# An mLSTM, soft-MoE and SoLU kernel: gate terms kept in one run for each head and chunk, and weights fetched from ScalarE's queue

## The reference, cut to what matters

```
m_new  = maximum(f_gate[t] + m, i_gate[t])
f_stab = exp(f_gate[t] + m - m_new);  i_stab = exp(i_gate[t] - m_new)
C = f_stab * C + i_stab * outer(v[t], k[t]);  n = f_stab * n + i_stab * k[t]
y[t] = sigmoid(o_gate[t]) * (C @ q[t]) / maximum(|n . q[t]|, 1)
```

## Time and profile before

| | |
|---|---|
| median of 3 runs | 301.03 us (300.47 to 301.7) |
| the profiled execution, its own time | 300.29 us |
| its span in the profile | 298.5 us |
| mean granted TensorE clock over the span | 0.966 |
| TensorE matmul busy | 277.6 us, 93% |
| VectorE, ScalarE, GpSimd busy | 223.2, 212.1, 152.1 us |
| moved by DMA | 50.35 MB |

### The profile page before, as it was taken

How to read it: one execution, slowest core, us unless ns; L and a number is a source line. 1 busy time by engine, 2 the same in 40 slices (tenths; PEclk the granted TensorE clock), 3 DMA queues, 4 the chain that set the end, 5 groups by cost and what they waited for, 6 DMA issues and landing times.

```text
span 298.5 us, 10417 instructions
## 1 busy us (share of the span) xinstructions
PE 277.6 (93%) x3909; PEld 189.0 (63%) x3934; DVE 223.2 (75%) x459; ACT 212.1 (71%) x675; POOL 152.1 (51%) x210
## 2 busy tenths in 40 slices
PE   8796999999989999999899989999999999999985
PEld 3464888888878888886315434666566666656653
DVE  7668557988878989875671048888988989889872
ACT  8675557786878787854117114798988989889895
POOL 2348447666767674455200602365464654646544
PEclk9999559999999999999989999999999999999999
DMA  5998985979989897999497000001010110101102
GB/s 144 270 274 194 350 298 159 319 211 307 311 247 303 225 317 213 369 393 379 161 431 315 0 2 0 2 24 45 24 47 22 47 46 24 46 25 46 45 24 88
DMA packets 22345, 50.35 MB, mean 169 GB/s; under 512 B 5944, under 2 KB 15128, under 8 KB 20120
## 3 DMA queue, kind: packets, MB, share of 16 engines
q1 hardware_dynamic: 22296, 49.70, 50.5%
HBM read 44.04 MB, written 4.18 MB: 162 GB/s over the span
## 4 chain that ended last, share of the span: by engine, by line
PE 50%; ACT 20%; issue 9%; DVE 9%; SPq 6%; DMA 3%; POOL 2%; DVEq 0%; POOLq 0%; ACTq 0%
PE ps L691 7%; ACT ring L1295 7%; ACT ring L1283 7%; PE ps L706 6%; PE ps L1014 6%; PE ps L901 4%; DVE ring L1609 4%; PE ps L937 3%; PE ps L786 3%; PE ps L773 2%; ACT ring L1262 2%; PE ps L676 2%; DMA kept_dram<-ring 2%; PE ps L977 2%; DMA arena<-kept_dram 1%
## 5 line engine op out<-in xcount | busy, mean ns | idle before, releaser
L1014 PE MATMUL ps<-arena,ring 128*128 128x321 bf16 x576 | 87.9, 301 | 1.0 <-DVE ring L1649 1.0
L633 POOL TENSOR_TENSOR ring<-ring 128x1024 bf16<-128x1024 f32 x23 | 43.6, 1896 | 59.7 <-DVE ring L1649 53.9
L1014 PEld LDWEIGHTS ps<-arena,ring 128*128 128x128 bf16 x576 | 54.3, 98 | 26.0 <-issue 4.4
L1295 ACT ACTIVATE ring<-ps,ring 128x256 f32<-128x256 f32 x96 | 44.2, 472 | 18.2 <-DVE ring L1666 18.2
L1324 DVE TENSOR_TENSOR ps<-ps,arena 128x512 f32<-128x512 f32 x48 | 33.2, 699 | 21.7 <-PE ps L691 15.0
L1083 ACT ACTIVATE arena<-ps 128x512 f32<-128x512 f32 x48 | 28.5, 593 | 20.3 <-PE ps L677 16.9
L1283 ACT ACTIVATE ring<-ring 128x256 bf16<-128x256 f32 x96 | 38.7, 420 | 0.0
L547 POOL TENSOR_TENSOR arena<-arena,sig 128x320 f32<-128x320 f32 x24 | 19.6, 815 | 34.4 <-DVE arena L1356 30.1
L1103 ACT CAST arena<-ps 128x512 bf16<-128x512 f32 x48 | 27.8, 582 | 8.4 <-DVE ps L1324 8.4
L1609 DVE TENSOR_REDUCE ring<-ps 128x4 f32<-128x1024 f32 x24 | 29.4, 1225 | 5.1 <-PE ps L977 4.7
L1333 DVE TENSOR_TENSOR arena<-ps,arena 128x512 bf16<-128x512 f32 x48 | 32.5, 684 | 0.9 <-ACT arena L1103 0.5
(11 more groups left out here) (206 smaller groups left out, 597.9 us busy)
## 6 DMA issues: line engine op xcount, KB each, us to landing
ring<-w_dram SPq DMA_DIRECT2D x8, 1280.0 KB, 9.5
arena<-kv_dram SPq DMA_DIRECT2D x24, 324.0 KB, 6.1
arena<-qkT_dram SPq DMA_DIRECT2D x48, 160.0 KB
arena<-w_dram SPq DMA_DIRECT2D x5, 1280.0 KB, 8.0
sig<-o_gate_dram SPq DMA_DIRECT2D x24, 160.0 KB, 6.4
sig<-w_dram SPq DMA_DIRECT2D x3, 1280.0 KB, 8.8
out_dram<-ring SPq DMA_DIRECT2D x24, 160.0 KB, 1.8
wout_words<-w_out_dram SPq DMA_DIRECT2D x1, 1280.0 KB, 7.7
```

What stands on the lines that cost most here:

```text
L633: pool.tensor_tensor(low(TT[i % 3]), TT[i % 3], high(TT[i % 3]), ALU.subtract) \
L1014: last = pe.matmul(o, low(words) if part == 2 else high(words), w[:, j, 0:DM + 1], start=(part == 0 and j == 0), stop=(part == 2 and j == ...
L1295: last = act.activation(ET[i % 2][:, group(g)], h_banks(i)[:, group(g)], ACT.Exp, bias=nmx[i % 2][:, g:g + 1], accum_out=sums[i % 4][:, 0, ...
```

## The change

There are two parts.

First, `kept` is viewed as `terms_kept[chunk and head, term, position]`, so that a head's six rows of a chunk are one run of 1536 bytes. The write of chunk 1 moves ahead of the `onehot` transfers, of `far["i"]` and of `mfar`, and the rows of all four tiles of chunk 1 are read by four transfers (`load_second_chunk`) in the place of sixteen, ahead of the load of tile 4. The mask and the `onehot` transfer are each split in two, so that they leave out the partitions that the terms fill. The far terms are written by one transfer in the place of four. On ScalarE the four copies of step 0 come ahead of the spreading of `own_head`.

Second, w1[0] to w1[7] and w_out are issued by ScalarE in its steps 3 to 20 and no longer by SyncE.

```diff
@@ SyncE
-                sp.dma_start(moving[PICK:ROWS, b * H:(b + 1) * H, :],
-                             kept[0:G3].rearrange("(r h) t -> r h t", r=3)[:, b * H:(b + 1) * H, cols]) \
-                    .then_inc(l_in[b], 16)
+                sp.dma_start(moving[PICK:ROWS, b * H:(b + 1) * H, :],
+                             terms_kept[heads_of, 0:3, :].rearrange("h r t -> r h t")).then_inc(l_in[b], 16)
...
+            def load_second_chunk():
+                second = slice(BH, FAR)
+                sp.wait_ge(s["rows_kept"], 16)
+                sp.dma_start(moving[PICK:ROWS, :, :], terms_kept[second, 0:3, :].rearrange("h r t -> r h t")) \
+                    .then_inc(s["near_rows_in"], 16)
+                for r in range(3):
+                    sp.dma_start(fixed[r * HALF:(r + 1) * HALF, :, :],
+                                 terms_kept[second, 3 + r, :].rearrange("(g j) t -> j g t", j=HALF)) \
+                        .then_inc(s["near_rows_in"], 16)
+            terms_kept = kept.rearrange("n (r t) -> n r t", r=6)
             load_tile(2)
             load_tile(3)
-            sp.dma_start(moving...(causal[:, :])...)                          # masks_in
-            far["f"], far["i"]; wait m_ready; mfar x4; wait ident_copied
-            sp.dma_start(fixed[:, :, :], again(onehot[:, :], 1, 2 * B)).then_inc(s["onehot_in"], 16)
-            sp.wait_ge(s["second_rows"], 6)
-            sp.dma_start(kept[:, :, L:2 * L], near_terms[BH:FAR, :, :])       # rows_kept
+            for rows in (slice(ROWS + 1, P), slice(ROWS, ROWS + 1)):
+                sp.dma_start(moving[rows]...(causal[rows, :])...)             # masks_in
+            sp.dma_start(far["f"], f_gate[FAR:NC * BH, :]).then_inc(s["far_in"], 16)
+            sp.wait_ge(s["second_rows"], 6)
+            sp.dma_start(terms_kept[BH:FAR], near_terms[BH:FAR, :, :]).then_inc(s["rows_kept"], 16)
+            sp.wait_ge(s["ident_copied"], 2)
+            for rows in (slice(PICK, ROWS + 1), slice(ROWS + 1, P)):
+                sp.dma_start(fixed[rows, :, :], again(onehot[rows, :], 1, 2 * B)).then_inc(s["masks_in"], 16)
+            sp.dma_start(far["i"], i_gate[FAR:NC * BH, :]).then_inc(s["far_in"], 16)
+            wait m_ready; mfar x4; wait own_ready
+            sp.dma_start(moving[0:PICK]..., again(own_head[:, :], 1, 2 * B)).then_inc(s["masks_in"], 16)
+            load_second_chunk()
             for i in range(B, NT):
...
-                if i == B:  (own_head, then load_row(4), behind load_tile(4))
-                if i == 2 * B + 1:
-                    sp.dma_start(wout_words[:, :, :], ...).then_inc(s["wout_in"], 16)
-                for e in w1_behind.get(i, ()):
-                    load_w1(e)
+                if i == 2 * B - 1:
+                    sp.wait_ge(s["far_ready"], 6)
+                    sp.dma_start(terms_kept[FAR:NC * BH], far_terms[:, :, :]).then_inc(s["rows_kept"], 16)
@@ TensorE, exponents
-                    pe.wait_ge(l_in[b], 64 * c)
-                    pe.wait_ge(s["picks_in"], 16)
+                    if i == B:
+                        pe.wait_ge(s["masks_in"], 80)
+                        pe.wait_ge(s["near_rows_in"], 64)
+                    await_loaded(pe, l_in[b], 64 * (c - 1))
@@ ScalarE, pieces(0): spread_heads() behind the four second_copy
+            w1_in_step = {3: (0,), 5: (1,), 8: (2,), 10: (3,), 13: (4,), 16: (5,), 19: (6,), 20: (7,)}
+            def weights(n):
+                for e in w1_in_step.get(n, ()):
+                    fetch_w1(e)
+                if n == 6:
+                    act.dma_start(wout_words[:, :, :], w_out.rearrange("(j p) n -> p j n", p=P)) \
+                        .then_inc(s["wout_in"], 16)
                 ...
                     finish_gate(n)
                     pieces(n)
+                    weights(n)
```

More of the change, by code:

```diff
@@ L391, in load_row @@
                     sp.dma_start(fixed[r * HALF:(r + 1) * HALF, 2 * b:2 * b + 2, :],
[L392 removed]
+                                 terms_kept[heads_of, 3 + r, :].rearrange("(f j) t -> j f t", j=HALF)) \
+                        .then_inc(l_in[b], 16)
+            def load_second_chunk():
[7 more added lines that the diff above has]
+                        .then_inc(s["near_rows_in"], 16)
@@ L394, in _ @@
+            terms_kept = kept.rearrange("n (r t) -> n r t", r=6)
             load_tile(2)
             load_tile(3)
-            sp.dma_start(moving.rearrange("p (g j) t -> p g (j t)", j=HALF), again(causal[:, :], 1, 2 * B)) \
-                .then_inc(s["masks_in"], 16)
-            for name, g in (("f", f_gate), ("i", i_gate)):
-                sp.dma_start(far[name], g[FAR:NC * BH, :]).then_inc(s["far_in"], 16)
+            for rows in (slice(ROWS + 1, P), slice(ROWS, ROWS + 1)):
+                sp.dma_start(moving[rows].rearrange("p (g j) t -> p g (j t)", j=HALF), again(causal[rows, :], 1, 2 * B)) \
+                    .then_inc(s["masks_in"], 16)
@@ L403, in _ @@
                     .then_inc(s["far_m_in"], 16)
-            sp.wait_ge(s["ident_copied"], 2)
-            sp.dma_start(fixed[:, :, :], again(onehot[:, :], 1, 2 * B)).then_inc(s["onehot_in"], 16)
-            sp.wait_ge(s["second_rows"], 6)
-            sp.dma_start(kept.rearrange("(r h) t -> h r t", h=BH)[:, :, L:2 * L], near_terms[BH:FAR, :, :]) \
-                .then_inc(s["rows_kept"], 16)
-            def load_w1(e):
-                if e == own_slot - 1:
-                    sp.wait_ge(s["coefs_ready"], 2)
-                    sp.wait_ge(s["far_words"], 3)
-                if e == own_slot:
-                    sp.wait_ge(s["far_m_in"], 16 * (NC - NEAR))
-                if e == own_slot + 2:
-                    sp.wait_ge(s["coefs_ready"], 4)
-                if e < RING:
-                    sp.dma_start(ring[:, e, :], w1[e]).then_inc(s["w1_first_in"], 16)
-                else:
-                    sp.dma_start(w1_place(e), w1[e]).then_inc(s["w1_late_in"], 16)
-            w1_behind = {5: (0,), 6: (1,), 12: (2,), 14: (3,), 17: (4,), 20: (5,), 23: (6, 7)}
-            assert sorted(e for es in w1_behind.values() for e in es) == list(range(E))
+            sp.wait_ge(s["own_ready"], 2)
+            sp.dma_start(moving[0:PICK].rearrange("p (g j) t -> p g (j t)", j=HALF), again(own_head[:, :], 1, 2 * B)) \
+                .then_inc(s["masks_in"], 16)
+            load_second_chunk()
             for i in range(B, NT):
                 sp.wait_ge(s["e_done"], 2 * (i - B) + 2)
-                if i % B or i > 2 * B:
+                if i > 2 * B:
                     load_row(i)
@@ L433, in _ @@
                 load_tile(i)
[L434 to L441 removed]
                 if i == 2 * B:
[L443 removed]
+                    sp.wait_ge(s["rows_kept"], 32)
                     load_row(i)
@@ L1173, in pieces, with fetch_w1 @@
                     far_exponentials()
+            def fetch_w1(e):
+                if e == own_slot - 1:
+                    act.wait_ge(s["coefs_ready"], 2)
+                    act.wait_ge(s["far_words"], 3)
+                if e == own_slot:
+                    act.wait_ge(s["far_m_in"], 16 * (NC - NEAR))
+                if e == own_slot + 2:
+                    act.wait_ge(s["coefs_ready"], 4)
+                if e < RING:
+                    act.dma_start(ring[:, e, :], w1[e]).then_inc(s["w1_first_in"], 16)
+                else:
+                    act.dma_start(w1_place(e), w1[e]).then_inc(s["w1_late_in"], 16)
+            w1_in_step = {3: (0,), 5: (1,), 8: (2,), 10: (3,), 13: (4,), 16: (5,), 19: (6,), 20: (7,)}
+            assert sorted(e for es in w1_in_step.values() for e in es) == list(range(E))
+            def weights(n):
[4 more added lines that the diff above has]
+                        .then_inc(s["wout_in"], 16)
             def scale_w_out(j):
```

25 lines of the change are left out of this document (6 added, 19 removed).

## The result

The changed kernel is slower. Its median is 315.49 us (307.68 to 320.04, 4 runs) against 301.37 for the kernel before beside it (300.47 to 302.77, 4 runs); the ratio is 1.031, interval 1.023 to 1.038. The forecast was 294.7 us and faster. A second group of runs gave 313.89 (306.24 to 322.36, 4 runs) against 301.82, ratio 1.017, interval 1.006 to 1.027. Some executions of every kernel run in a slower state of the chip: the ratios leave these out and the medians don't, so where the two differ the ratio decides, and the profiled executions of the first group, of parts 1 and 2 alone, of tile 4's load first, of w1[2] to w1[7] early from ScalarE and of w1[0], w1[1] and w1[3] alone are such ones. The profiled executions are one of 320.04 us (span 318.2) and, of the second group, one of 309.2 us (span 307.4).

A forecast was written before the change was run, and what follows sets the result against it. TensorE bounds attention, with late rows costing a wait and two half-clock steps. Terms -1.1 - 5.65 - 0.45 + 0.7 + 0.2 = -6.3 from 300.29 give 294.0, plus 0.74 for the median: 294.7 us, range 292.8 to 299.4.

The forecast's parts named there:

- The write issued at 14.7 to 15.2 us: SyncE's queue: chunk 1's terms' write goes out some 3.7 us earlier than its old 18.67 us.
- Landed at 21.8: Chunk 1's terms' write reaches memory at 21.8 us, the later of two bounds, as it waits its turn behind the mask.
- Reads landed at 27.5, queries at 27.6 to 28.9: Tile 4's data arrive then; rows could come until 28.0 and queries until 28.6 us without cost.
- Two slow steps at full clock, -5.65: Steps of tiles 4 and 5: 7.61 and 7.60 us fall to 4.80 and 4.75, saving 5.65 us.
- The next step, -0.45: The step behind the two slow ones, 5.69 us at clock 0.91, falls to 5.25, saving 0.45 us.
- ScalarE's nine issues, +0.7: Issuing w1 and w_out from ScalarE: six exposed issues at 0.12 us each add 0.7 us.
- The far terms, +0.2: far["i"] and maxima go out about 2.5 us later; VectorE's scan behind GpSimd may wait, adding 0.2 us.
- the 1.1 us of the first one: Start of tile 4's scores: at 28.6 us and not at 29.69, saving 1.1 us.
- The weights themselves cost no more to move: DMA engines: 1.28 MB fetches beside tile loads add no time, the share being 0.86 to 1.05 already.
- The second: Rival at tile 4: w1[0] beside late queries, TensorE's wait and slow steps stay; 301.0 to 301.7 us, chance 0.12.
- The first: Rival at tile 4: rows, queries or clock partly miss, half of the 6.3 us gain remains; 297.5 us, chance 0.10.
- The third, ScalarE blocked: Rival on ScalarE: six exposed issues of 1.84 us delay the exponentials, costing 11 us; 305 us, chance 0.06.

The follow-up runs named there:

- part 1 alone: Kernel before with the terms' new layout and order, w1 and w_out still in SyncE's queue: 304.37 us against 301.82, ratio 0.996.
- part 2 alone: Kernel before with all nine fetches of w1 and w_out issued by ScalarE: 309.44 us against 301.82, ratio 1.012.
- tile 4's load first: New terms layout and order without the ScalarE fetches, tile 4's load issued ahead of the rows' read: 307.63 us against 302.21, no ratio.
- w1[2] to w1[7] early from ScalarE: Kernel before with these six fetched by ScalarE in steps 8, 10, 13, 16, 19 and 20: 311.19 us against 301.89, ratio 1.027.
- w1[0], w1[1] and w1[3] alone: Three kernels, each the one before with one fetch from ScalarE, in steps 3, 5 and 10: 303.66, 301.73 and 301.55 us; ratios 1.011, 0.999, 1.011.
- far gates first: New terms layout without ScalarE fetches, far["i"] and maxima ahead of the terms' write, tile 4's load ahead of the reads: 305.83 us against 302.09, ratio 1.010.
- the clock held by extra work: Kernel before with eight extra matmuls in step 4 and two in each of steps 5 to 7: 301.5 us against 302.09, ratio 1.005.
- the six later ones: Kernel before with w1[2] to w1[7] fetched earlier: from ScalarE 311.19 us, ratio 1.027; from SyncE 307.44 us, ratio 1.017.
- w1[0] in step 7: Changed kernel with w1[0] fetched in step 7 and not in step 3: 312.82 us, ratio 1.029.
- the six in their old places: Kernel before with w1[2] to w1[7] issued by ScalarE in the steps where SyncE issued them: 303.95 us against 303.53, ratio 1.003.
- w_out fetched early: Kernel before with only w_out issued by ScalarE, in step 6 and not behind tile 9's load: 304.58 us against 301.89, no ratio.

## Why the prediction was wrong, point by point

- *The write issued at 14.7 to 15.2 us.* Nearly: 15.45. *Landed at 21.8.* Wrong, and the first step that failed: 23.9, no earlier than before. The prediction set the write just behind `far["f"]`, at the 21.7 us at which this landed before. It did land just behind it, but `far["f"]` itself was issued at 13.92 and took 9.2 us, until 23.1, 1.4 us later than before. The mask's two transfers, put at 1.2 us, took 2.52 to issue, and `far["i"]` 3.29 for the 1.00 of before. In all nine profiled executions with part 1's order the engines moved 221 to 253 GB/s from 13 to 21 us and the write took 8.4 to 10.6 us; in the eleven without it they are 256 to 310 GB/s and 3.9 to 6.9 us. With the far gates first, `far["i"]` was issued at 14.36 us, as before (14.28), and still landed in 11.9 us and not 7.9, and the one edit ahead of it in the queue is the split of the mask. That split is thus the suspect, but no run has it alone, so the cause stays open.
- *Reads landed at 27.5, queries at 27.6 to 28.9.* Wrong: the last read took 6.29 us from 25.48, until 31.8, and the scores of tile 4 began at 34.45. About 1 us of it was there with part 1 alone (30.85 against 29.69), and 3 us came with w1[0] in step 3 (31.70 without, 34.45 and 35.36 with). The row of 4.3 us that the prediction read as tile 6's is of tile 5's load; 8.4 us were measured.
- *Two slow steps at full clock, -5.65.* Wrong twice. The wait did not go, so the steps stayed slow (7.61 and 7.61, then 9.03). And with the clock held by extra work, the time was the same (301.5 against 302.09, ratio 1.005): this term was not to be had in the sum in any kernel tried, as data came late further on. This is the costliest error, since it was nine tenths of the gain.
- *The next step, -0.45.* It fell with the one before.
- *ScalarE's nine issues, +0.7.* Right. An issue takes 0.33 to 0.40 us and lies under the scaling; scaling to exponential is 0.60 us in the step with an issue and 0.48 in the earlier trace rows:

```profile
64.76 0.56 ACT L1111 ACTIVATE sig<-sig,half 128x320 f32<-128x320 f32 x1
64.82 0.35 ACTq L1177 DMA_DIRECT2D ring<-w_dram  x1
65.36 0.60 ACT L1075 ACTIVATE arena<-ps 128x512 f32<-128x512 f32 x1
```

- *The far terms, +0.2.* Mis-sized. GpSimd waited 3.40 us for the maxima, not the 2 that the prediction named as its limit, and VectorE 2.14 us for GpSimd, with tile 3's remainders behind it in its list. These ended 2.3 us later than the 28.44 on which the prediction built its start of tile 4. So this term alone took away the 1.1 us of the first one and made a wait of over 2 us, without any late rows; the prediction gave VectorE's scan "some tenths" and did not carry them on to the remainders behind it.
- *"The weights themselves cost no more to move ... the DMA share of these steps is 0.86 to 1.05 already."* This sentence was the deepest mistake. The share was read as proof that nothing changes. It left little room: to fetch 1.28 MB two tiles earlier takes it from the rows and queries of those tiles. The nine fetches were counted for their issue alone. Measured by the ratios, the six later ones cost some 8 us from ScalarE and some 5 from SyncE.
- *The rivals.* The second named the place, the mechanism and the trigger rightly (w1[0] beside the queries, which stand behind all of chunk 1's rows; the queries over 1.5 us late), and priced it at no change, because it counted one wait in exchange for another. The first has a slip: half of the 6.3 us leaves 297.9 and not 297.5. The third, ScalarE blocked, did not occur in the changed kernel. No rival was slower by way of the DMA engines, so the side that came true had 0.06.

The sum of the two parts is not settled. In one group part 1 alone has the ratio 0.996, part 2 alone 1.012 and the changed kernel 1.017 (1.006 to 1.027). The parts together would give 1.008, inside that interval, but the first group of the changed kernel has 1.031. The loss behind tile 23 in the first profile (176.36 against 171.45) goes with half clock at 135 to 159 us and is absent in the second (170.19); why an execution falls there and another not stays open. That the "issue" waits of 1 to 4 us at tile 10 are waits for data is shown by name in three kernels, which name the queries (part 1 alone, 1.39 us; far gates first, 1.74; w1[0] in step 7, 1.42); in the others it is argued from the same place and from landings of 10.1 us. None of the kernels tried beats the one before: the lowest medians are those of the held clock (301.5) and of w1[3] alone (301.55), and their ratios (1.005 and 1.011) say the same or slightly slower; the fastest run of before in that group was 296.69. The lowest ratio is that of part 1 alone, 0.996, and its interval reaches 1.001.

## What to carry to other kernels

When the DMA engines are nearly full in a stretch (0.84 to 1.05 here), treat them as a possible bound behind the visible one: work out for each transfer that moves earlier which tile's data it now stands beside, and what is saved in TensorE's steps before that stretch as worth nothing until the data also come earlier. A full share by itself is not yet a wait: with w_out fetched early, the stretch of 60 to 70 us was 0.88 busy and lost nothing. What counts is what stands ahead of the next tile's data. A half-clock stretch may cover for transfers that would be late otherwise, so ask what is late next when it goes. A big fetch from a second queue doesn't wait its turn behind small urgent ones, so its moment has to be kept clear of them.

## What the runs showed of the hardware

- A fetch of 1.28 MB in a second queue can stop a queue of small transfers almost wholly: 94.3% of the engines' time against 0.8% for two microseconds, and in another run a small transfer issued 0.4 us behind such a fetch landed 11.2 us later, at the end of a wait of 8.95 us. The Trainium skill, "DMA: Bandwidth & Descriptors", section Queues, rings and completion order, says that an engine takes turns between its queues and drains a whole packet of several descriptors before it changes. The rows don't test this. From 27 to 29 us 15 packets of the small transfers stand against 75 of w1[0], from 26 to 28 us 196 against 53, and how many were ready is not shown.
- The same page's section Issuing engines are not separate DMA queues says that another issuing engine saves issue time alone. This case agrees in the time when the moment is kept (303.95 us against 303.53, ratio 1.003, interval 0.998 to 1.009).
- Two fetches issued by ScalarE in one step are not hidden. In the kernel with the six in their old places, ScalarE's timeline in step 21, and TensorE's behind it:

```profile
119.61 1.31 ACTq L1186 DMA_DIRECT2D arena<-w_dram  x2
121.05 0.60 ACT L1082 ACTIVATE arena<-ps 128x512 f32<-128x512 f32 x1 [0.88 <-DVE ps L1345]
```

```profile
123.87 1.16 PE L690 MATMUL ps<-arena 40*128 40x128 f32 x16 [1.18 <-DVE arena L1354]
```

  The pair took 1.31 us where one takes 0.35, and the exponential behind it came at 121.05, 0.13 us behind the pair's end. The row puts the idle time down to VectorE, but that instruction had ended at 120.50. TensorE idled 1.18 us, and from 126.7 to 130.1 us it was at 1.2 GHz. This is the third rival's mechanism, at one place.
- Eight extra matmuls in a wait of 2.5 us kept the granted clock at 2.4 GHz until 42 us; then it fell until 56 us, and the steps of tiles 6 and 7 took 7.8 and 8.4 us in the place of those of tiles 4 and 5.
- The issue of a transfer is not of fixed price: three reads of rows took 0.96 us as a rule, and 3.79 with w1 in flight.
- The same busy share doesn't mean the same rate: at 1.04 in both kernels, the engines moved 296 GB/s before and 243 after between 13 and 21 us.
